# Batch 0 of a fused attention, Fourier mix and two MLPs: where the low halves of the weights, the sums of x and the first visits of batch 1 stand

## The chip, the cores and the metric

One core of a Trainium2 chip runs the whole program. The metric is the device time of one execution in microseconds (us). Before the change the median of three runs was 900.11 us (899.06 to 900.23).

## What is computed

Three layers follow one another on 4 batches of 768 tokens with 384 channels, all in float32:

```python
for t in range(S):                                   # attention layer, 8 heads of 48, per batch
    state = alpha[:, :, t, :, None] * state + einsum('bhd,bhe->bhde', k[:, :, t], v[:, :, t])
    y[:, :, t] = einsum('bhd,bhde->bhe', q[:, :, t], state)
...
u = x + real(fft(fft(x, axis=1), axis=2))            # Fourier layer, tokens then channels
un = (u - mean(u)) / sqrt(var(u) + 1e-6)
x = u + relu(un @ w_ch1) @ w_ch2                      # MLP 1: 384 -> 1536 -> 384
...
u = x + (relu(x.T @ w_tok1) @ w_tok2).T               # token mix
out = u + relu(u @ w2_ch1) @ w2_ch2                   # MLP 2
```

## The kernel before

**Numbers in two parts.** Every large product is exact to float32 by splitting each operand into a high part (a rounding copy, `fp32r`) and a low part (the difference). `three` issues high x high, high x low and low x high, at lines 1388 to 1390. A low part of an activation or a weight is a subtraction on DVE or POOL, and the high part is a copy on ACT.

**Stages.** The attention of batch 0 runs alone (`visit(0, k)`, k from -2 to 23: 4 units of two heads, 6 chunks of 128 tokens each). Its Fourier part and the first three normalised tiles follow (`tail(0, h)`, h from 31 to 47), again alone. Then the loop over b runs MLP 1 of batch b in 48 half steps h: an even h has `mlp_in` (9 matmuls of 384 columns into bank 0 or 1), an odd one `mlp_out` (9 matmuls into banks 2 to 4). Between them stand, for batch b+1, one visit in each half step up to h = 30 that isn't in `PAUSES`, and then the tail from h = 31. "MLP 0" below is this loop at b = 0. The second part of the program (token mix and MLP 2 of all batches) isn't touched.

**What a visit does.** For chunk k of batch a: PE computes the scores of chunk k+1 (L1402 in batch 0, L1406 later) and the state's product (L1415), after DVE has masked the scores before (`at`, L1049) and updated the state (`st`, L903 or L906). Then it applies `at` and the decayed state to chunk k (L1425 or L1430, L1434) and transposes the keys of chunk k+2 (L1395). DVE also prepares chunk k+3: suffix scan `suf` (L919), reciprocal, prefix scan (L931), and POOL multiplies keys and queries by them (L569, L579) and decays the state (L592). ACT copies `qz`, `krt`, `x` and `dec`. Once per unit DVE reduces the decays twice (`extreme`, L893).

**What a tail does.** `fold`: DVE adds and subtracts the two token halves of x (`x_sum`, tmp, L1054), then folds channel c with channel 384-c into xf (L1094 to L1102). `split_x` makes xh (ACT, L742) and xl (DVE, L1114). PE multiplies three flips of x (L1475), then `f1` 0 to 5, then after `split_g` (gh on ACT, gl on DVE L1118) the second transform `f2_v`, `f2_u` and `f2_middle`. `copy_flipped` (ACT, L729) and `first_edge_rows` (ACT, L734) copy the flips. From the product v, ACT makes vs (L756), DVE and POOL build u (L1127, L621, L629), and `fourier_u` (DVE, L1142) adds the product u. Statistics and un (L1193 on DVE) follow, then PE transposes un (`norm`, L1534), and nh and nl (L775, L1199) are the input of the MLP. `fill` (L1587) issues matmuls whose result nobody reads; a call of 1 shows as 2 in the trace.

**The weights.** `w_ch1` is 3 items of 128 rows (0 to 2), `w_ch2` 3 items of 4 row groups (3 to 5). Each item has two halves. The raw copies arrive on SP's queue, ACT makes the high part (`weight_hi`, L672), POOL or DVE the low one (`weight_lo`, L558 or L1278). One counter for the highs and one for the lows fix the order: before the change it is item by item. In it POOL makes halves 0 to 2 inside the attention, 3 to 5 once `xlo` is done, 6 and 7 in the first two visits of MLP 0; DVE makes 8 to 11 at h = 9, 11, 15, 17. PE waits for all of `w_ch1` before MLP 0 and for item 3 before `mlp_out(0)` at h = 5, where it also waits for all of `fourier_u` (counter `s_ua` at 10), because the result banks 2 to 4 hold Fourier products.

Nothing is planned at run time: the tables of half steps and the order of the calls in `tail` and `visit` of each engine are the whole order. Each engine runs its own list in that order, and semaphores make it wait.

Of the kernel before, what the change touches and what calls it, by code (L numbers as in the profile page):

```python
# [10 lines left out]
P = 128  # L11
# [41 lines left out]
EDGE_AT = 36  # L53
FILL_TO, FILL_COL = 5, 384
VISIT = dict(zip([h for h in range(31) if h not in PAUSES], range(-2, STEPS)))
# [9 lines left out]
LATE_NORM_AT = {9: 3, 13: 4, 20: 5}  # L65
# [25 lines left out]
def program(nc, qka, v, v_sizes, w_ch1, w_ch2, w_tok1, w_tok2, w2_ch1, w2_ch2, dft, cs, mask_in, ident_in, flip_in, col_in, out):  # L91
# [189 lines left out]

    def raw_sem(i):

        return s_raw[i % 2], 16 * (i // 2 + 1)

    def norm_bank(b, t):

        return bank[((7, 6, 4) if b == 0 else (6, 7, 6))[t] if t < 3 else 6]
# [105 lines left out]
    def f1_bank(a, i):  # L394

        return bank[5 + i % 3 if a else (5, 6, 7, 1, 5, 6)[i]]

    def v_bank(a, j):

        return bank[(5, 5, 7)[j] if a else (5, 2, 5)[j]]  # L400

    def u_bank(a, j):

        return bank[(6, 6, 5)[j] if a else (6, 3, 2)[j]]
# [15 lines left out]
    with nc.Block() as block:  # L420
# [131 lines left out]
        def _(pool):  # L552

            def weight_lo(i):
                i, half = i // 2, i % 2
                pool.wait_ge(s_whi, 2 * i + half + 1)
                src, hi, lo = halves(i, half)
                pool.tensor_tensor(lo, src, hi.bitcast(F32), ALU.subtract).then_inc(s_wlo, 1)  # L558
# [81 lines left out]
            pool.wait_ge(s_xlo, 2 * KT)  # L640
            for i in range(len(LOW_AT), LOW_F1):
                weight_lo(i)
            for a in range(B):
                if a:
                    for k in range(-2, STEPS):
                        visit(a, k)
                        if a == 1 and k < 0:
                            weight_lo(LOW_F1 + k + 2)
                fourier_v(a)
                if a:  # L650
                    fourier_v_last(a)
# [3 lines left out]
                if a == 0:  # L655
                    fourier_v_last(a)
# [9 lines left out]
        def _(act):  # L666

            def weight_hi(i):
                i, half = i // 2, i % 2
# [46 lines left out]
            def visit(a, k):  # L716
                for h in range(2 if a and (a, k) != (1, -2) else 0):
                    attn_qz(a, k + 2, h)
# [17 lines left out]
            def split_x(a, part):  # L736
                act.wait_ge(s_fold, a * 8 + (4, 8)[part])
                for i in range(part * KT, (part + 1) * KT):
                    t = f1_tile(i)
# [4 lines left out]
            def split_g(a, i):  # L744
                act.wait_ge(s_gp, a * (2 * KT) + i + 1)
                if i == 0:
                    act.wait_ge(s_fold, a * 8 + 8)
# [76 lines left out]
            for b in range(B):  # L824
                for h in range(SLOTS):
# [4 lines left out]
                    if b == 0 and h == 2:  # L830
                        for i in range(2):
                            attn_qz(1, 0, i)
# [10 lines left out]
                    if b + 1 < B:  # L843
                        if h in VISIT:
                            visit(b + 1, VISIT[h])
# [42 lines left out]
        def _(dve):  # L888
# [172 lines left out]
            def visit(a, k):  # L1061
# [11 lines left out]
                if k in (FLAG + 2, FLAG + 3):  # L1073
                    early_sum(a, k - FLAG - 2)
                if k == (FLAG - 2 if a else TEST_AT):
                    range_test(a)

            def fold(a):
# [7 lines left out]
                fold_direct(a, 0)  # L1086
                fold_rest(a, 0)
                x_sum(1, slice(EARLY, DM)).then_inc(s_xs, 1)

            def fold_direct(a, part):  # L1090

                r = slice(part * KT, (part + 1) * KT)
                dve.wait_ge(s_xs, 2 * a + part + 1)
                dve.tensor_tensor(xf[:, r, 1:192], tmp[:, r, 1:192], tmp[:, r, 383:192:-1], ALU.add).then_inc(s_fold, 1)  # L1094

            def fold_rest(a, part):
# [47 lines left out]
            def fourier_middle(a):  # L1144
# [4 lines left out]
                dve.tensor_tensor(u[0:1, 1, 0:n], bank[7][0:1, 0:n], x[0:1, 3, 0:n], ALU.add).then_inc(s_ua, 1)  # L1149
                dve.tensor_tensor(u[0:1, 1, n:DM], bank[7][0:1, n - 2:0:-1], x[0:1, 3, n:DM], ALU.add  # L1150
# [50 lines left out]

            def tail(a, h):
                if h == SUMS_AT:
                    fold(a)
                if h == SUMS_AT + 1:
                    split_x(a, 0)
                    fold_direct(a, 1)
                    split_x(a, 1)
                    fold_rest(a, 1)
                    split_x(a, 2)  # L1210
                if h == SUMS_AT + 2:
                    for i in range(KT, 2 * KT):
                        split_x(a, i)
                if 0 <= h - F1_AT < 2 * KT:
                    split_g(a, h - F1_AT)
                if h == F1_AT + 2 and a:
# [547 lines left out]
```

## Time and profile before

| | before |
|---|---|
| median of 3 runs | 900.11 us |
| the profiled execution | 900.5 us |
| its span, first to last instruction | 898.7 us |
| PE busy | 880.7 us, 98% |
| DVE busy | 456.3 us, 51% |
| ACT busy | 302.3 us, 34% |
| POOL busy | 195.8 us, 22% |
| granted TensorE clock, mean | 0.992 |

The span plus 1.8 us of start and end is the time of that execution, which is 0.4 us above the median. A granted clock of 1.00 is the 2.4 GHz level and 0.50 the 1.2 GHz level. A busy share is a mean over stages: the attention and Fourier part of batch 0 (the first 75 us) has no MLP work beside it, while from 75 us on MLP matmuls fill PE.

### The profile page before, as it was taken

The numbers are of one execution on the slowest core, as the hardware profiler recorded it, in microseconds if no ns is written. First come the engines' busy times: TensorE is split into PE (matmuls) and PEld (weight loads), VectorE is DVE, ScalarE is ACT, GpSimd is POOL, SyncE is SP. The second block draws the span as 40 slices with busy tenths as digits, with TensorE's granted clock in tenths as the row PEclk, the third lists the DMA queues.
The fourth block names the chain that finished last, engine by engine and source line by source line (L and its number), as shares of the span: only waits on it lengthen the run. The fifth ranks groups of instructions, "written<-read, shape, count | busy, mean of one in ns | idle before, by whom it ended". The sixth has DMA issues, their size and how long they took to land.

```text
span 898.7 us, 14545 instructions
## 1 busy us (share of the span) xinstructions
PE 880.7 (98%) x5378; PEld 851.5 (95%) x5378; DVE 456.3 (51%) x1085; ACT 302.3 (34%) x795; POOL 195.8 (22%) x326
## 2 busy tenths in 40 slices
PE   9996999999999999999999999999999999999998
PEld 6786999999999999999999999999999999999998
DVE  6778877658776479776552244221422142214221
ACT  2864555424544325554223242211221122112111
POOL 4754343013333023331104312000200020002000
PEclk9989999999999999999999999999999999999999
DMA  8942120040220131300054011000100010000000
GB/s 214 320 135 81 43 78 2 27 119 27 61 60 28 39 81 45 99 4 28 1 198 136 27 54 54 1 27 27 53 0 26 26 53 0 26 26 0 0 27 27
DMA packets 15002, 51.23 MB, mean 57 GB/s; under 512 B 1489, under 2 KB 6385, under 8 KB 13009
## 3 DMA queue, kind: packets, MB, share of 16 engines
q1 hardware_dynamic: 14368, 47.35, 17.4%
q0 software_dynamic: 576, 3.15, 1.0%
q8 instruction: 31, 0.51, 0.2%
q14 instruction: 27, 0.21, 0.1%
HBM read 41.07 MB, written 9.44 MB: 56 GB/s over the span
## 4 chain that ended last, share of the span: by engine, by line
PE 90%; DVE 5%; ACT 2%; issue 2%; POOL 0%; DVEq 0%; POOLq 0%
PE bank L1388 13%; PE bank L1389 13%; PE bank L1390 13%; PE pair L1388 12%; PE pair L1389 12%; PE pair L1390 12%; PE pair L1406 3%; PE bank L1425 3%; PE bank L1434 2%; PE pair L1415 2%; PE bank L1581 1%; PE bank L1534 1%; ACT tested L712 1%; PE bank L1430 1%; PE bank L1395 1%
## 5 line engine op out<-in xcount | busy, mean ns | idle before, releaser
L1255 DVE SCALAR_TENSOR_TENSOR hl<-bank,hh 128x384 fp32r<-128x384 f32 x192 | 106.8, 557 | 326.4 <-ACT hh L804 326.4
L804 ACT ACTIVATE hh<-bank 128x384 fp32r<-128x384 f32 x192 | 94.2, 491 | 352.7 <-PE bank L1390 352.7
L1388 PE MATMUL pair<-w2h,hh 128*128 128x384 f32 x288 | 101.9, 354 | 2.0 <-issue 2.0
L1388 PE MATMUL bank<-nh,w1h 128*128 128x384 f32 x288 | 102.7, 356 | 0.0
L1388 PE MATMUL bank<-u2h,w3h 128*128 128x384 f32 x288 | 96.9, 337 | 0.8 <-DVE u2l L1344 0.8
L1389 PE MATMUL pair<-w2l,hh 128*128 128x384 f32 x288 | 97.5, 338 | 0.0
L1390 PE MATMUL pair<-w2h,hl 128*128 128x384 f32 x288 | 97.4, 338 | 0.0
L1389 PE MATMUL bank<-nl,w1h 128*128 128x384 f32 x288 | 97.3, 338 | 0.0
L1388 PE MATMUL pair<-w4h,hh 128*128 128x384 f32 x288 | 97.2, 338 | 0.0
L1390 PE MATMUL bank<-nh,w1l 128*128 128x384 f32 x288 | 97.2, 337 | 0.0
L1389 PE MATMUL pair<-w4l,hh 128*128 128x384 f32 x288 | 97.0, 337 | 0.0
L1390 PE MATMUL bank<-u2h,w3l 128*128 128x384 f32 x288 | 96.5, 335 | 0.0
L1389 PE MATMUL bank<-u2l,w3h 128*128 128x384 f32 x288 | 96.5, 335 | 0.0
L1390 PE MATMUL pair<-w4h,hl 128*128 128x384 f32 x288 | 96.2, 334 | 0.0
L662 POOL TENSOR_TENSOR u<-u,x2l 128x384 f32<-128x384 f32 x24 | 23.6, 1016 | 274.9 <-DVE u L1365 274.9
L569 POOL TENSOR_TENSOR qkap<-qkap,suf 112x128 f32<-112x128 f32 (+1 forms) x81 | 39.8, 491 | 121.1 <-DVE suf L919 112.0
L686 ACT ACTIVATE qz<-qkap 48x128 f32<-48x128 f32 x144 | 44.2, 307 | 48.0 <-POOL qkap L579 45.5
L1388 PEld LDWEIGHTS pair<-w2h,hh 128*128 128x128 f32 x288 | 54.7, 190 | 2.3 <-issue 2.2
L1388 PEld LDWEIGHTS bank<-u2h,w3h 128*128 128x128 f32 x288 | 54.1, 188 | 2.1 <-issue 2.1
L1388 PEld LDWEIGHTS bank<-nh,w1h 128*128 128x128 f32 x288 | 54.8, 190 | 0.7 <-issue 0.2
L1389 PEld LDWEIGHTS bank<-nl,w1h 128*128 128x128 f32 x288 | 54.7, 190 | 0.4
L1389 PEld LDWEIGHTS pair<-w2l,hh 128*128 128x128 f32 x288 | 54.7, 190 | 0.0
(201 smaller groups left out, 1843.0 us busy)
## 6 DMA issues: line engine op xcount, KB each, us to landing
qkap<-qka SPq DMA_DIRECT2D x15, 1011.5 KB, 7.5
vt<-v SPq DMA_DIRECT2D x16, 288.0 KB, 8.0
raw_a<-w_ch SPq DMA_DIRECT2D x6, 768.0 KB, 12.1
mid<-u SPq DMA_DIRECT2D x8, 576.0 KB, 2.8
raw_b<-w_ch SPq DMA_DIRECT2D x6, 768.0 KB, 6.3
out<-u SPq DMA_DIRECT2D x8, 576.0 KB, 2.8
xr<-mid SPq DMA_DIRECT2D x7, 576.0 KB, 3.9
raw_t<-w_tok SPq DMA_DIRECT2D x2, 768.0 KB, 6.0
```

Source lines behind the costliest of these rows:

```text
L569: pool.tensor_tensor(keys.rearrange("p (c n) -> p c n", n=P), keys.rearrange("p (c n) -> p c n", n=P), after.rearrange("p (c n) -> p c n", ...
L662: pool.tensor_tensor(u2[:, t, :], u2[:, t, :], x2l[:, t, :].bitcast(F32), ALU.add).then_inc(s_u2, 1)
L686: act.activation(qz[head_rows(h), k % 2, h, :], q_of(a, k, head_rows(h)), ACT.Copy).then_inc(s_qz, 1)
L804: act.activation(hh[:, s % 4, :], bank[s % 2][:, 0:HALF], ACT.Relu).then_inc(s_hhi, 1)
L1255: dve.scalar_tensor_tensor(out=hl[:, s % 4, :], in0=bank[s % 2][:, 0:HALF], scalar=0.0, in1=hh[:, s % 4, :].bitcast(F32), op0=ALU.max, op1 ...
L1388: pe.matmul(out_ap, wh, rh, start=first, stop=False)
L1389: pe.matmul(out_ap, wh, rl, start=False, stop=False)
L1390: return pe.matmul(out_ap, wl, rh, start=False, stop=last)
L1406: return pe.matmul(score_bank(a, k)[:, 0:2 * P], k_of(a, k), qz[0:PR, k % 2, :, :].rearrange("p h t -> p (h t)"), start=True, stop=True)
L1415: return pe.matmul(kv_of(a, k), krt[:, s % 2, 0:PR], vt[unit_buffer(a, k // NC)][:, k % NC, :], start=True, stop=True)
L1425: mm = pe.matmul(y[:, h * D:(h + 1) * D], at[:, k % 2, h, :], vb[:, c, h * D:(h + 1) * D], start=h == 0, stop=c == 0 and h == 1)
L1434: mm = pe.matmul(y, q_of(a, k), dec[0:PR, k % 3, :], start=False, stop=True)
```

## The change

- The sums of x in batch 0 are made unit by unit, 6 pieces of 96 channels in visits 19 to 22, instead of two sums over 288 channels in visits 20 and 21.
- The halves of the weights are taken in another order (`WEIGHT_ORDER`): the first halves of w_ch1, then item 3, then the second halves of w_ch1. POOL makes only two lows (visits 17 and 19); DVE makes one at h = 33 of the tail and nine in MLP 0. PE's waits follow: 3 lows before MLP 0, 8 at h = 12, and 5, 10, 12 before the three parts of w_ch2.
- In MLP 0 the visits of batch 1 go from h = 5 to 30 without a pause. In MLPs 1 and 2 the pauses are 0, 1, 11, 15, 21, and the late normalisations stand at 11, 15, 21 everywhere (before: 9, 13, 20).
- The fold is cut in pieces: xf columns 1 to 127 first, then the edge columns, 128 to 254, and 256 to 383, with `split_x` between them. This holds for all batches.
- In batch 0's tail: other banks for f1, f2 and norm; ACT copies the flips and edge rows at h = 35, behind three `split_g`, instead of ahead of the first; `fill` at h = 44 is 10 instead of 6; POOL's last four products come before its preparation of batch 1; and DVE's `extreme`, prefix scan and last `fourier_u` move from the tail's end to h = 1 of MLP 0.

```diff
-PAUSES = (0, 1, 9, 13, 20)
+WEIGHT_ORDER = ((0, 0), (1, 0), (2, 0), (3, 0), (3, 1), (0, 1), (1, 1), (2, 1), (4, 0), (4, 1), (5, 0), (5, 1))
+PAUSES = ((0, 1, 2, 3, 4), (0, 1, 11, 15, 21), (0, 1, 11, 15, 21))
-FILL = {44: 6, 46: 4}
+FILL = {44: 10, 46: 4}
-HI_AT = (16, 18, 20, 21)
-HI_FOLD, HI_V, HI_MLP = 7, 10, {4: 10, 6: 11}
-LOW_AT = (17, 19, 21)
-LOW_F1 = 6
-LATE_LOW_AT = {9: 8, 11: 9, 15: 10, 17: 11}
+HI_AT = (16, 18, 20)
+HI_FOLD, HI_V, HI_MLP = 6, 9, {4: 9, 6: 10, 8: 11}
+LOW_AT = (17, 19)
+LOW_F1 = 2
+LOW_MLP = {0: (3, 4), 6: (5,), 8: (6,), 9: (7,), 10: (8,), 11: (9,), 13: (10,), 16: (11,)}
+EARLY_AT = {19: (0,), 20: (1, 2), 21: (3,), 22: (4, 5)}
-EDGE_AT = 36
+FLIPS_AT = 35
-LATE_NORM_AT = {9: 3, 13: 4, 20: 5}
+LATE_NORM_AT = {11: 3, 15: 4, 21: 5}
...
 (POOL)
-            pool.wait_ge(s_xlo, 2 * KT)
-            for i in range(len(LOW_AT), LOW_F1):
-                weight_lo(i)
...
-                if a:
-                    fourier_v_last(a)
+                fourier_v_last(a)
                 if a + 1 < B:
                     prep_k(a + 1, 0, 1)
                     prep_q(a + 1, 0, 1)
-                if a == 0:
-                    fourier_v_last(a)
 (ACT, split_x and tail)
-                act.wait_ge(s_fold, a * 8 + (4, 8)[part])
+                    act.wait_ge(s_fold, a * 10 + (2, 4, 5, 8, 10, 10)[i])
...
+                if a == 0 and h == FLIPS_AT:
+                    copy_flipped(0)
+                    first_edge_rows()
 (DVE)
+                if a == 0:
+                    for i in EARLY_AT.get(k, ()):
+                        dve.wait_ge(s_ext, 2 * NU)
+                        dve.wait_ge(s_x, NC * (i // 2 + 1))
+                        x_sum(i % 2, slice(i // 2 * PW, (i // 2 + 1) * PW))
...
                 if h == SUMS_AT + 1:
                     split_x(a, 0)
-                    fold_direct(a, 1)
+                    fold_high(a, 0)
                     split_x(a, 1)
-                    fold_rest(a, 1)
+                    late_sum(a)
                     split_x(a, 2)
+                    fold_middle(a, 1)
+                    fold_edges(a, 1)
                 if h == SUMS_AT + 2:
-                    for i in range(KT, 2 * KT):
-                        split_x(a, i)
+                    fold_low(a, 1)
+                    split_x(a, 3)
+                    fold_high(a, 1)
+                    split_x(a, 4)
+                    split_x(a, 5)
...
+                    if b == 0:
+                        for p in LOW_MLP.get(h, ()):
+                            weight_lo(p)
+                    if b == 0 and h == 1:
+                        next_unit(1)
+                        fourier_u(0, 4, 2, 0)
+                        fourier_u(0, 4, 2, 1)
 (PE)
-            pe.wait_ge(s_wlo, 2 * KT)
...
+                        if b == 0 and s in (0, NF // 2):
+                            pe.wait_ge(s_wlo, 8 if s else 3)
...
-                            pe.wait_ge(s_wlo, 2 * (KT + 1 + (s - 2) // FG))
+                            pe.wait_ge(s_wlo, {2: 5, 6: 10, 10: 12}[s])
```

First place: ACT in the tail of batch 0, from the last copy of x (`x<-bank`) to the first vs. Before the change:

```order
L692 ACTIVATE x<-bank 128x96 x2
L672 ACTIVATE w1h<-raw_a_113 128x768 x2
L672 ACTIVATE w2h<-raw_a_114 128x4x192
L742 ACTIVATE xh<-xf 128x3x128 x6
L729 ACTIVATE u_90<-pair 128x384 x3
L748 ACTIVATE gh<-pair 128x194
L748 ACTIVATE gh<-bank 128x2x192
L748 ACTIVATE gh<-bank 128x192
L734 ACTIVATE u_90<-x 1x2x384
L748 ACTIVATE gh<-bank 128x2x192
```

With the change:

```order
L693 ACTIVATE x<-bank 128x96 x2
L673 ACTIVATE w2h<-raw_a_114 128x4x192 x2
L673 ACTIVATE w1h<-raw_a_111 128x768
L743 ACTIVATE xh<-xf 128x3x128 x6
L749 ACTIVATE gh<-pair 128x194
L749 ACTIVATE gh<-bank 128x2x192
L749 ACTIVATE gh<-bank 128x192
L730 ACTIVATE u_90<-pair 128x384 x3
L735 ACTIVATE u_90<-x 1x2x384
L749 ACTIVATE gh<-bank 128x2x192
```

The three copies of the flips moved behind three `gh`, and next to the edge rows, in front of the fourth `gh`.

Second place: DVE from the end of the tail (batch 1's first suffix scan) to the first masked scores of batch 1. Before the change:

```order
L919 SCALAR_TENSOR_TENSOR suf<-qkap_57,zeros 112x128 [waits visit_done,qka_loaded0]
L925 RECIPROCAL inv<-suf 112x1 [waits suffix_done]
L893 TENSOR_REDUCE ext<-qkap_57 112x1 [waits qka_loaded0] x2
L931 SCALAR_TENSOR_TENSOR qkap_57<-qkap_57,inv,zeros 112x128 [waits inverse_ready,ext_ready]
L1142 TENSOR_TENSOR u_90<-u_90,pair 128x2x193 [waits u_done,v_added]
L1142 TENSOR_TENSOR u_90<-u_90,pair 128x2x191
L1255 SCALAR_TENSOR_TENSOR hl<-bank,hh 128x384 [waits hidden_hi] x2
```

With the change:

```order
L914 SCALAR_TENSOR_TENSOR suf<-qkap_57,zeros 112x128 [waits visit_done,qka_loaded0]
L920 RECIPROCAL inv<-suf 112x1 [waits suffix_done]
L1283 SCALAR_TENSOR_TENSOR hl<-bank,hh 128x384 [waits hidden_hi]
L1306 TENSOR_TENSOR w2l<-raw_a_114,w2h 128x4x192 [waits weight_lo,weight_hi] x2
L888 TENSOR_REDUCE ext<-qkap_57 112x1 [waits qka_loaded0] x2
L926 SCALAR_TENSOR_TENSOR qkap_57<-qkap_57,inv,zeros 112x128 [waits inverse_ready,ext_ready]
L1158 TENSOR_TENSOR u_90<-u_90,pair 128x2x193 [waits u_done,v_added]
L1158 TENSOR_TENSOR u_90<-u_90,pair 128x2x191
L1283 SCALAR_TENSOR_TENSOR hl<-bank,hh 128x384 [waits hidden_hi] x2
```

The reductions, the prefix scan and the last `fourier_u` moved behind the first `hl` and behind the two lows of item 3, which POOL made before.

## Rows read from the trace of the kernel before

**Rows 1.** The page: busy time, share of the span and instructions
```profile
PE 880.7 (98%) x5378; PEld 851.5 (95%) x5378; DVE 456.3 (51%) x1085; ACT 302.3 (34%) x795; POOL 195.8 (22%) x326
```

**Rows 2.** PE's waits, whole span: total us, times, longest
```profile
PE bank L1395 <- POOL qkap L569: 3.3, 1, 3.3
PE bank L1534 <- DVE un L1193: 2.0, 4, 1.2
PE pair L1388 <- issue: 2.0, 1, 2.0
PE bank L1430 <- DVE at L1049: 1.5, 1, 1.5
```

**Rows 3.** Stretches: width, PE busy, PEld, DVE, ACT, POOL busy, granted clock, DMA
```profile
48.30:55.20 6.90, 6.90 (x22) 5.43 (x23) 4.65 (x12) 5.14 (x10) 2.91 (x2) 0.51 0.42 133
72.10:75.00 2.90, 2.83 (x18) 2.51 (x19) 2.33 (x6) 1.75 (x5) 0.00 (x0) 1.00 0.57 155
83.20:85.70 2.50, 2.50 (x9) 2.50 (x10) 2.50 (x4) 1.21 (x4) 2.19 (x2) 0.50 0.00 0
89.40:92.60 3.20, 3.14 (x10) 3.17 (x11) 0.95 (x3) 0.62 (x2) 1.24 (x3) 0.50 0.00 0
93.90:115.40 21.50, 21.29 (x141) 20.57 (x140) 20.02 (x57) 12.86 (x40) 8.31 (x19) 1.00 0.24 63
```

**Rows 4.** DVE in order of time, visit 20: start, us, line, what
```profile
44.76 2.58 DVE L1054 TENSOR_TENSOR tmp<-x 128x864 f32<-128x864 f32 x1
```

**Rows 5.** POOL in order of time, visit 19
```profile
44.60 1.82 POOL L558 TENSOR_TENSOR w1l<-raw_a,w1h 128x768 fp32r<-128x768 f32 x1
```

**Rows 6.** ACT in order of time, tail of batch 0
```profile
53.91 1.35 ACT L742 ACTIVATE xh<-xf 128x384 fp32r<-128x384 f32 x3
...
58.25 1.23 ACT L729 ACTIVATE u<-pair 128x384 f32<-128x384 f32 x3
...
60.16 0.83 ACT L734 ACTIVATE u<-x 1x768 f32<-1x768 f32 x1
61.40 0.52 ACT L748 ACTIVATE gh<-bank 128x384 fp32r<-128x384 f32 x1 [0.41 <-PE bank L1390]
```

**Rows 7.** PE in order of time, tail of batch 0
```profile
55.74 0.55 PE L1388 MATMUL pair<-dfth,xh 128*128 128x194 f32 x1
...
63.19 0.35 PE L1388 MATMUL pair<-csh,gh 128*128 128x194 f32 x1
...
68.16 2.77 PE L1587 MATMUL bank<-mask,ident 128*128 128x256 f32 x12
72.17 0.87 PE L1534 MATMUL bank<-ident,un 128*128 128x128 f32 x6 [1.24 <-DVE un L1193]
...
74.88 0.41 PE L1388 MATMUL bank<-nh,w1h 128*128 128x384 f32 x1
```

**Rows 8.** PE in order of time, start of MLP 0
```profile
78.10 0.26 PE L1395 MATMUL bank<-ident,qkap 112*128 112x112 f32 x1
...
89.46 0.66 PE L1388 MATMUL pair<-w2h,hh 128*128 128x384 f32 x1 [2.01 <-issue]
...
115.43 0.42 PE L1388 MATMUL bank<-nh,w1h 128*128 128x384 f32 x1
```

**Rows 9.** DVE in order of time, MLP 0
```profile
75.18 1.79 DVE L893 TENSOR_REDUCE ext<-qkap 112x1 f32<-112x768 f32 x2
...
80.22 1.02 DVE L1142 TENSOR_TENSOR u<-u,pair 128x386 f32<-128x386 f32 x2 [2.72 <-POOL u L629]
...
95.16 1.45 DVE L1156 BATCH_NORM_STATS2 stats<-u 128x6 f32<-128x384 f32 x3
...
104.31 0.55 DVE L1255 SCALAR_TENSOR_TENSOR hl<-bank,hh 128x384 fp32r<-128x384 f32 x1
...
110.28 0.42 DVE L1049 TENSOR_TENSOR at<-pair,mask 128x256 f32<-128x256 f32 x1 [0.50 <-PE pair L1415]
...
111.96 0.93 DVE L1278 TENSOR_TENSOR w2l<-raw_a,w2h 128x768 fp32r<-128x768 f32 x1
```

More of the change, by code:

```diff
@@ L52 @@
 TEST_AT = 20
-EDGE_AT = 36
+FLIPS_AT = 35
 FILL_TO, FILL_COL = 5, 384
-VISIT = dict(zip([h for h in range(31) if h not in PAUSES], range(-2, STEPS)))
+VISITS = [dict(zip([h for h in range(31) if h not in pauses], range(-2, STEPS))) for pauses in PAUSES] + [{}]
 SUMS_AT = 31
@@ L552, in _, with weight_lo @@
         def _(pool):
[L554 to L557, printed above, removed]
+            def weight_lo(p):
+                pool.wait_ge(s_whi, p + 1)
+                src, hi, lo = halves(*half_at(p))
                 pool.tensor_tensor(lo, src, hi.bitcast(F32), ALU.subtract).then_inc(s_wlo, 1)
@@ L716, in visit @@
             def visit(a, k):
-                for h in range(2 if a and (a, k) != (1, -2) else 0):
+                for h in range(2 if a else 0):
                     attn_qz(a, k + 2, h)
@@ L734, in first_edge_rows, with split_x @@
                 act.activation(us[0][0:1, 3:6:2, :], x[0:1, 5:3:-1, :], ACT.Copy).then_inc(s_rows, 1)
-            def split_x(a, part):
-                act.wait_ge(s_fold, a * 8 + (4, 8)[part])
-                for i in range(part * KT, (part + 1) * KT):
-                    t = f1_tile(i)
+            def split_x(a, step):
+                for i in ((0, 1), (2,), (3, 4, 5))[step]:
+                    t, part = f1_tile(i), i // KT
+                    act.wait_ge(s_fold, a * 10 + (2, 4, 5, 8, 10, 10)[i])
                     m = slice(t * P, (t + 1) * P)
@@ L1200, in norm_split, with next_unit @@
                                   nh[:, :, cols].bitcast(F32), ALU.subtract).then_inc(s_nlo, 1)
+            def next_unit(a):
+                for i in range(2):
+                    extreme(a, 0, i)
+                prep_prefix(a, 0)
             def tail(a, h):
@@ L1245, in tail @@
                         prep_inverse(1, 0)
-                    for i in range(2):
-                        extreme(a + 1, 0, i)
-                    prep_prefix(a + 1, 0)
-                if h == 46:
+                    else:
+                        next_unit(a + 1)
+                if h == 46 and a:
                     for i in range(2):
@@ L1309, in _ @@
                         hidden(b, s)
-                    if b + 1 < B and h in VISIT:
-                        visit(b + 1, VISIT[h])
+                    if b == 0:
[5 more added lines that the diff above has]
+                        fourier_u(0, 4, 2, 1)
+                    if h in VISITS[b]:
+                        visit(b + 1, VISITS[b][h])
                     if h == LATE_STATS_AT:
@@ L1334, in _ @@
             for half in range(2):
-                weight_lo(NA + NW4, half)
+                weight_lo(2 * (NA + NW4) + half)
                 split_x2(0, half)
@@ L1338, in _ @@
             for half in range(2):
-                weight_lo(NA + NW4 + 1, half)
+                weight_lo(2 * (NA + NW4 + 1) + half)
             def split_u2(b, t):
@@ L1513, in f2_u @@
                     pe.wait_ge(s_ua, a * UA + 2)
-                elif j == 2:
+                elif j == 2 and a:
                     pe.wait_ge(s_vc, a * 3 + 2)
```

107 lines of the change are left out of this document (54 added, 53 removed).

## The prediction

> **What bounds the kernel now.** I read the page first, then PE's waits, then the stretches with the granted clock, then the timelines of the places that the change touches. PE is busy 880.7 of 898.7 us [rows 1], so a gain can only come from PE's waits and from matmuls at the low clock level. The list of waits has four places of a microsecond or more [rows 2], all ahead of 90 us: one of 1.5 us in the attention of batch 0 (masked scores from DVE), 1.2 us of the 2.0 us of un, 3.3 us in MLP 0 (POOL's keys), and 2.0 us "issue", which is PE's wait for the lows of item 3. A wait also costs clock. After the 1.5 us wait PE ran for 6.9 us at a granted 0.51 (1.2 GHz), after the 3.3 us one 2.5 us at 0.50 and after the 2.0 us one 3.2 us at 0.50; after the 1.24 us one it stayed at 1.00 [rows 3, 7]. Eighteen MLP matmuls take 78.10 - 74.88 = 3.22 us at full clock, 0.179 each [rows 7, 8]; nine are 1.6 us, and about 2.9 us at half, so a low stretch costs about 1.3 us. All in all 80 to 93 us holds some 8 us that aren't work, and 48 to 55 us another 5.
>
> **Step 1, the sums of x.** DVE's sum in visit 20 took 2.58 us [rows 4]. It had started 0.16 us after POOL's low of visit 19, which took 1.82 us [rows 5]; it ended 0.92 us after it. So DVE stood still while POOL subtracted, and PE waited 1.5 us for the scores behind [rows 2]. The change removes POOL's low of visit 21, but not this one, and puts two pieces of the sum into visit 20. They meet the same low. A piece is a third of 288 channels, about 0.4 us, and POOL's decays, which stand ahead of the low, may slip by as much behind the piece of visit 19. I take +0.3 us for the path. Afterwards the flips run on PE as before, so the earlier folds gain nothing: f1(0) starts 0.3 us later than 55.74. Bounds: -2.9 us if the pieces get through and the clock stays up, +0.5 us if two waits on POOL follow each other.
>
> **Step 2, the tail's fold and ACT.** On ACT the two last highs ahead of xh are three, as before, so xh(0) stays at about 53.9 [rows 6]. Behind it the chain is longer: the pieces stand between the xl's, and the second sum too. Counting 0.47 us for each piece of 384 elements (a fold half or an xl), 0.4 us for the sum, 0.6 us for the middle and edges, and 0.45 us for each xh [rows 6] that waits for its piece, xh(5) ends near 60.0. ACT then does three gh (0.8 us), the three flips (1.23 us) and the edge rows (0.83 us) [rows 6]: the fourth gh starts near 62.6, where it was at 61.40. Its gl and the fifth gl end near 64.05, and f2_v(0), which stood at 63.19 [rows 7], waits for them: +0.87 us. The low at h = 33 (0.93 us, as in [rows 9]) lies on DVE between two gl that wait for ACT anyway: nothing. Of the 0.87 us PE wins 0.25 back at f2_u(0), which waited before. Bounds 0 (ACT keeps up) and +1.3.
>
> **Step 3, the filler.** Twelve filler matmuls took 2.77 us, and PE then waited 1.24 us for un [rows 7]. Twenty take 4.62 us. PE arrives at 68.16 + 0.3 + 0.62 + 4.62 = 73.7; un is there at about 72.17 + 0.3 + 0.87 = 73.3. So norm starts 1.5 us later than at 72.17, and MLP 0 at 74.88 + 1.5 = 76.4. The new banks cost and bring nothing, since PE had no wait between 64.2 and 68.16.
>
> **Step 4, the first half steps of MLP 0.** DVE finishes its first suffix scan, waits for hl(0) (ready about 79.3, since mlp_in(0) ends at 78.0 and ACT and DVE take 0.5 each [rows 9]), then does two lows (2 x 0.86), two reductions (1.8), a prefix scan (0.5) and the last fourier_u (1.0) [rows 9]: 84.3. PE has done three mlp_in by 81.1 and stands before mlp_out(0), which waits for just that fourier_u. **The wait of 3.3 us is there again, with another name.** One low stretch follows, 1.3 us. What is gone is the 2.0 us for POOL's lows [rows 8] and the second low stretch, 1.3 to 1.6 us: the lows of item 3 are ready at 81.0. The wait before fourier_u (2.72 us, DVE for POOL's u [rows 9]) is gone from DVE too.
>
> **Step 5, the dense stretch.** mlp_out(0) and the first transpose take PE to about 87.6, where h = 6 begins. For h = 6 to 13 PE took 21.5 us before [rows 3]. It now has two visits more (1.3 each) and one normalisation less (0.4): 21.5 + 2.6 - 0.4 - 0.2 (the un wait) = 23.5 us. DVE was busy 20.02 us of the same stretch [rows 3]. It now has six lows in it instead of two (+3.5), two visits more (1.68 each, from the scores at 110.28 to the low at 111.96 [rows 9]: +3.4), but no statistics (1.45 and 0.45 after it [rows 9]: -1.9) and one split less (-0.5): 24.5 us. **DVE becomes the bound here**, and I count 24.7 us with the joints: PE waits about 0.5 us before the scores in h = 9, 11 and 12. That ends at 112.3. Before, PE was there at 115.43 [rows 8], with a visit and a normalisation more behind it (1.7 us). So 112.3 + 1.7 = 114.0 against 115.4: **-1.4 us**, with steps 1 to 4 in it. From h = 14 on DVE has 2.2 us a half step against PE's 2.9 and catches up.
>
> **Step 6, MLPs 1 and 2.** The late normalisation waits there for un once each, 2.0 - 1.24 = 0.8 us over three batches [rows 2, 7]; two half steps more take that away, 0.5 us outside MLP 0. In the tails of batches 1 to 3 the pieces of the fold stand on DVE with MLP matmuls over them; PE's needs come half steps later: nothing, and if the cover fails 0.3 us each.
>
> **The weights' new order** costs nothing as long as highs and lows stay ahead of PE: all second halves of w_ch1 by 100.3, needed at 106; item 4 by 107.8, needed at 109.3. That is the thinnest margin.
>
> Sum: -1.4 - 0.5 = -1.9 us. The profiled execution took 900.5 us, so 898.6; the median stood 0.4 us below it: **898.2 us**.
>
> **A rule weighed.** The 2.58 us of rows 4 is an engine that stands still for the rest of the other's instruction, not one that runs at half speed. The Trainium skill (SBUF — State Buffer, "Who interferes with whom") says that a DVE instruction with two SBUF inputs and a GpSimd instruction that reads SBUF exclude each other, and that the one issued first holds the ports to its end. By that rule POOL's low gets in ahead of a second piece wherever it was waiting, and the split gives no way past it; that is step 1 as I take it. Taken as a rate shared between both, the two pieces would end about a microsecond earlier and the sum would be near rival 1.
>
> **Rival 1, the pieces pass POOL.** If DVE keeps the ports for both pieces of visit 20, the scores come before PE asks, the 1.5 us wait and its 6.9 us at 0.51 go, and f1(0) is bound by xh instead of the flips, near 53.0. ACT's chain (step 2) gives some back: about 2.2 us better than my forecast, 896.0. For it: POOL's decays slip behind the first piece, so its low may start late. Against it: the observed order [rows 4, 5].
>
> **Rival 2, slower: DVE's lows starve the scores.** Place: h = 6 to 13. Each low also holds POOL's key and query products back, by up to its 0.93 us, and these hold the next scan and ACT's qz. If that adds 0.4 us to five half steps (+2.0) and PE's share of work there falls so far that the clock drops as it did after 1.5 us, twice at 1.4 us (+2.8), it ends at 898.2 + 4.8 = 903.0. It decides once a DVE half step with a low goes beyond about 3.4 us against PE's 2.9. For it: DVE was busy 93% of the stretch before [rows 3]. Against it: two lows were in it already and PE hardly waited.
>
> **Rival 3, nothing moves on balance.** The wait at mlp_out(0) grows to 5 us because hl(0) or the lows of item 3 come late, and eats the rest: about 900.1.
>
> **How the numbers follow.** A measurement of this kernel can tell about 0.2%, 1.8 us, from no change. Forecast 0.50, rival 1 0.22, rival 2 0.18, rival 3 0.10. The forecast's own bounds (steps 1 to 3, +-1.3 us) put a bit more than half of it below 898.3: 0.28 faster and 0.22 same. With rival 1 faster is 0.50, with rival 3 and a hundredth of rival 2 same is 0.33, slower 0.17. The range reaches from the middle of rival 1 (895.0, with its clock gain in full) to 901.6, which takes in rival 3 and the light end of rival 2.
>
> **What would show it.** Step 1: two tmp pieces in visit 20, the second over 1 us long, and PE's wait of about 1.5 us for `at` still in the list, with a clock of 0.5 until 55. Step 2: f2_v(0) waits for gl. Step 4: no "issue" wait of 2 us, but one of about 3.3 us before the first `pair<-w2h`, behind fourier_u, and one low stretch after it, not two. Step 5: DVE over 95% busy for some 25 us, and several waits of PE for `at` below 1 us. It is wrong if PE's total wait between 75 and 115 us falls below 2 us or stays over 8 us, or if the clock between 48 and 55 us is up.

## The result and the profile after

The changed kernel is slower: 901.83 us median of 8 runs (901.26 to 902.92), where the kernel before took 899.7 us beside it. The ratio is 1.0033, with a 95% interval of 1.002 to 1.0046, so the loss is 3.0 us. Medians are over all runs, a few of which took 912 to 920 us in a slower state that any of these kernels can fall into; the ratios, and the comparisons drawn below, leave those out. My prediction was 898.2 us with a range of 895.0 to 901.6, so it missed on the sign and, by 0.2 us, on the range.

| | before | after |
|---|---|---|
| the profiled execution | 900.5 us | 902.67 us |
| its span | 898.7 us | 900.9 us |
| PE busy | 880.7 us | 883.0 us |
| f1 of batch 0 begins | 55.74 | 56.35 |
| f2_v of batch 0 begins | 63.19 | 64.62 |
| MLP 0 begins | 74.88 | 76.32 |
| its first mlp_out | 89.46 | 84.37 |
| mlp_in of h = 14 | 115.43 (with a visit and a normalisation more behind it) | 114.07 |
| mlp_in of h = 24 | 143.30 | 144.11 |

From f1 on the rows are the start times, in us, of the first matmul named. At h = 24 both kernels have done the same number of visits and normalisations, so there the balance of batch 0 can be read: 0.81 us lost.

These two executions did not start alike. PE in order of time (start, us, line), first of the kernel before, then of the changed one:

```profile
1.48 8.36 PE L1581 MATMUL bank<-at 128*128 128x384 f32 x16 [1.48 <-DVE ones L1282]
9.67 0.26 PE L1395 MATMUL bank<-ident,qkap 112*128 112x112 f32 x1
...
38.95 0.41 PE L1415 MATMUL pair<-vt,krt 128*112 128x96 f32 x2 [0.45 <-ACT krt L679]
```

```profile
1.47 7.12 PE L1614 MATMUL bank<-at 128*128 128x384 f32 x16 [1.47 <-DVE ones L1310]
8.43 0.26 PE L1428 MATMUL bank<-ident,qkap 112*128 112x112 f32 x1
...
38.05 0.41 PE L1448 MATMUL pair<-vt,krt 128*112 128x96 f32 x2 [0.45 <-ACT krt L680]
```

The 16 matmuls ahead of the first product took 8.36 us in one and 7.12 us in the other, and 0.9 us of that difference is still there at 38 us. It isn't the change's: a second trace with the kernel before's code up to this point (the variant with the pauses moved, below) has 7.11 us there and stands at 38.02. So whoever subtracts one of these traces from the other finds the changed kernel 0.9 us better in batch 0 than it is. Added to the 2.2 us between the two spans, it comes near the 3.0 us of the ratio.

The page of the changed kernel, busy time by engine, answers to [rows 1]:

```profile
PE 883.0 (98%) x5386; PEld 853.1 (95%) x5386; DVE 461.4 (51%) x1103; ACT 303.6 (34%) x795; POOL 184.5 (20%) x320
```

PE's waits over the span (total us, times, longest us) answer to [rows 2]:

```profile
PE pair L1421 <- DVE u L1158: 3.1, 1, 3.1
PE pair L1439 <- ACT qz L687: 3.1, 3, 1.2
PE bank L1463 <- DVE at L1044: 1.5, 1, 1.5
PE pair L1439 <- DVE st L901: 0.7, 1, 0.7
PE bank L1421 <- DVE gl L1134: 0.6, 1, 0.6
```

The wait for POOL's keys and the "issue" wait are gone, and the wait for un with them. The 3.1 us for the last fourier_u and the 1.5 us for the masked scores are those I had forecast. The second line had 0.4 us before: three waits for ACT's qz. One of 0.77 us stands in MLP 0. The other two are in no step of my working. They are the next two rows, at half step 9 of MLP 1 and of MLP 2:

```profile
230.50 0.67 PE L1439 MATMUL pair<-qz,qkap 112*128 112x256 f32 x2 [1.17 <-ACT qz L687]
...
355.72 0.67 PE L1439 MATMUL pair<-qz,qkap 112*128 112x256 f32 x2 [1.18 <-ACT qz L687]
```

ACT in order of time, at the first of the two, shows what qz stands behind:

```profile
229.12 0.71 ACT L771 ACTIVATE un<-u,nrm 128x384 f32<-128x384 f32 x1 [2.02 <-DVE nrm L1202]
229.73 0.62 ACT L687 ACTIVATE qz<-qkap 48x128 f32<-48x128 f32 x2
```

ACT sits idle for 2.02 us in front of un, because DVE's Newton steps for the late normalisation end only at 229.08; qz comes behind un on the same queue. The kernel before has the same pair of ACT instructions with the same 2.02 us of idle time:

```profile
228.47 0.71 ACT L770 ACTIVATE un<-u,nrm 128x384 f32<-128x384 f32 x1 [2.02 <-DVE nrm L1186]
...
229.09 0.63 ACT L686 ACTIVATE qz<-qkap 48x128 f32<-48x128 f32 x2
```

It had a pause at half step 9, so PE had no visit there and asked for no qz. The change moves the pauses to 11, 15 and 21 and puts a visit exactly there.

### The profile page after: what moved, and what is told of

Read it like the earlier page. It is cut to its first block, busy times and chain, and to the rows that moved or that the text cites. A ratio compares the mean times of both kernels' runs of the same rounds, so it can differ in the third digit from the quotient of the medians.

```text
span 900.9 us, 14589 instructions
## 1 busy us (share of the span) xinstructions
PE 883.0 (98%) x5386; PEld 853.1 (95%) x5386; DVE 461.4 (51%) x1103; ACT 303.6 (34%) x795; POOL 184.5 (20%) x320
## 4 chain that ended last, share of the span: by engine, by line
PE 88%; DVE 4%; ACT 3%; issue 2%; DMA 1%; SPq 0%; POOL 0%; DVEq 0%; ACTq 0%
PE bank L1421 13%; PE bank L1422 13%; PE bank L1423 13%; PE pair L1421 12%; PE pair L1422 12%; PE pair L1423 12%; PE pair L1439 3%; PE bank L1458 3%; PE bank L1467 2%; PE pair L1448 1%; DMA qkap<-qka 1%; PE bank L1567 1%; ACT tested L713 1%; PE bank L1463 1%; PE bank L1428 1%
```

## The experiments

Each time is a median, each ratio is to the kernel before, measured beside it on the same chip, with its 95% interval. The runs of the kernel before spread over 896.8 to 901.2 us, so that single microseconds are read from the trace and the sum from the ratio.

**Pauses back.** In MLPs 1 and 2 alone, of the changed kernel:

```
-PAUSES = ((0, 1, 2, 3, 4), (0, 1, 11, 15, 21), (0, 1, 11, 15, 21))
+PAUSES = ((0, 1, 2, 3, 4), (0, 1, 9, 13, 20), (0, 1, 9, 13, 20))
-LATE_NORM_AT = {11: 3, 15: 4, 21: 5}
+LATE_NORMS = [{11: 3, 15: 4, 21: 5}] + [{9: 3, 13: 4, 20: 5}] * 3
```

> The changed kernel with the pauses of MLPs 1 and 2 and their late normalisations back at 9, 13, 20. Theory A, the half step h = 9 without a pause costs: ACT copies qz of the next visit behind the un that waits for DVE's Newton steps, and PE stood 1.17 and 1.18 us for it at 230.5 and 355.7 us, where the kernel before stood 0.30 and 0.27 us for un. Undone, the two waits go and the old ones return: 1.8 us faster than the changed kernel, about 900.0 us, 1.0013 of the kernel before. Theory B, the two waits only move within MLPs that DVE or ACT bound anyway: no difference, 1.0033 of the kernel before.

Measured: 899.72 us, ratio 1.0011 (1.0001 to 1.002), against 1.0033 of the changed kernel. Both qz waits are gone and the two of 0.3 us for un are back. By the ratios about two thirds of the loss lie here (2.0 of 3.0 us; the two intervals just meet at 1.002).

**The pauses alone, in the kernel before.**

```
+PAUSES_12 = (0, 1, 11, 15, 21)
-VISIT = dict(zip([h for h in range(31) if h not in PAUSES], range(-2, STEPS)))
+VISITS = [dict(zip([h for h in range(31) if h not in p], range(-2, STEPS))) for p in (PAUSES, PAUSES_12, PAUSES_12)] + [{}]
-LATE_NORM_AT = {9: 3, 13: 4, 20: 5}
+LATE_NORMS = [{9: 3, 13: 4, 20: 5}] + [{11: 3, 15: 4, 21: 5}] * 3
```

> The kernel before with one part of the change alone: in MLPs 1 and 2 the pauses at half steps 11, 15 and 21 and the late norms there, batch 0 as before. My theory (ACT's qz stands behind un, which waits for DVE's Newton steps, 0.9 us at h = 9 of each of two MLPs): slower by 1.8 us, ratio 1.002, and PE's chain shows two waits of about 1.2 us for qz near 229 and 354 us where 0.3 us for un stood. Rival (the forecast's own term: 0.5 us gained): ratio 0.9994. Second rival (the waits of the changed kernel came from its batch 0, by the phase at which batch 1 begins): ratio 1.000, no qz waits.

Measured: 901.21 us, ratio 1.0027 (1.0015 to 1.0039), slower, where no other part of the change is present. PE in order of time shows the same two waits:

```profile
226.82 0.67 PE L1407 MATMUL pair<-qz,qkap 112*128 112x256 f32 x2 [1.17 <-ACT qz L687]
...
352.18 0.67 PE L1407 MATMUL pair<-qz,qkap 112*128 112x256 f32 x2 [1.18 <-ACT qz L687]
```

Removing the part takes 2.0 us away by the ratios, adding it alone costs 2.4 us, and the trace has 1.8 us for it. The largest part of the loss is settled from both sides, and my forecast's own term (0.5 us gained) and the phase of batch 1 both fall.

**Sums of x whole again** (visits 20 and 21, as before):

```
-                if a and k in (FLAG + 2, FLAG + 3):
+                if k in (FLAG + 2, FLAG + 3):
-                if a == 0:
-                    for i in EARLY_AT.get(k, ()):
...
-                        x_sum(i % 2, slice(i // 2 * PW, (i // 2 + 1) * PW))
```

> The changed kernel with the sums of x whole again, 288 channels in visits 20 and 21; POOL's lows stay at visits 17 and 19. Theory A, the piece of visit 19 is what costs: DVE stood in it for 3.49 us behind four POOL instructions, the scores of chunk 21 came that late, and PE then ran 10.1 us at the low clock level instead of 6.9. Undone, DVE meets only POOL's second low, the low stretch falls back to about 7 us, f1(0) starts 1.2 us earlier against the attention: 1.2 us faster than the changed kernel, about 900.6. Theory B, only the number of POOL instructions counts and any sum there waits as long: no difference.

Measured: 900.61 us, ratio 1.0016 (1.0005 to 1.0026); this overlaps the changed kernel's interval. The profile of the same kernel is read from one more execution, of 901.67 us:

> The changed kernel with the sums of x whole again in batch 0 (visits 20 and 21, as before), looked at for its profile. My theory: no DVE instruction of a 0.45 us size then stands 3.49 us behind four GpSimd instructions; DVE's tmp in 41 to 47 us takes at most 2.5 us, the un wait and the wait at 46 us are gone or under 0.6 us, and f1 of batch 0 begins 0.5 to 1.5 us earlier than 56.35. Rival (the piece costs nothing, the clock alone differs between executions): f1 begins at 56.0 to 56.6 again, and a wait of 1 us or more stands at 44 to 47 us with the whole sums too. Time about 900.6.

DVE, POOL and PE of the changed kernel in order of time, around the piece of visit 19, first:

```profile
42.30 3.49 DVE L1049 TENSOR_TENSOR tmp<-x 128x288 f32<-128x288 f32 x1
...
46.27 0.81 DVE L1049 TENSOR_TENSOR tmp<-x 128x288 f32<-128x288 f32 x2
...
41.15 1.82 POOL L567 TENSOR_TENSOR w1l<-raw_a,w1h 128x768 fp32r<-128x768 f32 x1
42.95 0.76 POOL L601 TENSOR_SCALAR dec<-st,suf 48x48 f32<-48x48 f32 x2
43.68 1.79 POOL L567 TENSOR_TENSOR w1l<-raw_a,w1h 128x768 fp32r<-128x768 f32 x1
...
46.27 1.14 PE L1463 MATMUL bank<-vt,at 128*128 128x96 f32 x4 [1.46 <-DVE at L1044]
```

And the same engines with whole sums:

```profile
44.12 2.55 DVE L1049 TENSOR_TENSOR tmp<-x 128x864 f32<-128x864 f32 x1
...
43.94 1.81 POOL L567 TENSOR_TENSOR w1l<-raw_a,w1h 128x768 fp32r<-128x768 f32 x1
45.73 1.20 POOL L601 TENSOR_SCALAR dec<-st,suf 48x48 f32<-48x48 f32 x1
...
47.63 0.66 PE L1458 MATMUL bank<-vt,at 128*128 128x96 f32 x4 [1.47 <-DVE at L1044]
```

A piece of 0.4 us takes 3.49 us: it starts while POOL's first low runs and ends 0.3 us after the second, with two decays between them. The four other traces with this code in this place have 3.50 to 3.54 us. Two pieces with no low beside them take 0.81 us together. The whole sum waits only for one low: it got in directly behind it, and it was POOL's decay that took 1.20 us there instead of 0.39. But my theory of the price falls: PE's wait is still 1.47 us, one visit later. The rival had the wait right, and f1 wrong: it is 2.6 us earlier (53.71 against 56.35), and what differs there is the clock: after its 1.47 us wait this execution stayed at 1.00. Rows of stretches (width, busy time of PE, PEld, DVE, ACT, POOL, granted clock, DMA), changed kernel:

```profile
48.00:52.00 4.00, 4.00 (x19) 3.50 (x20) 1.80 (x6) 0.93 (x4) 0.54 (x1) 0.50 0.61 207
52.00:56.00 4.00, 4.00 (x9) 2.50 (x8) 2.81 (x8) 3.29 (x7) 0.00 (x0) 0.50 0.04 12
```

Whole sums, and there a low stretch further on, behind a wait of 1.67 us for gl at 62.92:

```profile
48.00:52.00 4.00, 3.33 (x20) 2.45 (x20) 2.67 (x8) 2.23 (x6) 0.94 (x1) 1.00 0.64 207
52.00:56.00 4.00, 3.52 (x20) 2.67 (x19) 2.87 (x8) 2.00 (x4) 0.00 (x0) 1.00 0.01 4
...
64.00:68.00 4.00, 4.00 (x25) 3.78 (x24) 3.46 (x10) 1.23 (x3) 0.45 (x1) 0.57 1.05 303
```

Of the 2.6 us little is left at MLP 0, which begins at 76.18 against 76.32: f2_v waits for DVE's gl (ACT's chain) and the clock falls there instead.

**No low on POOL in the attention.** All three of POOL's lows come after the last xl; none on DVE at h = 33:

```
-LOW_AT = (17, 19)
-LOW_F1 = 2
+LOW_AT = ()
+LOW_F1 = 3
...
-                    if a == 0 and h == F1_AT:
-                        weight_lo(LOW_F1)
...
+            pool.wait_ge(s_xlo, 2 * KT)
+            for i in range(LOW_F1):
+                weight_lo(i)
```

> The changed kernel with no low of the weights in the attention: POOL makes the first three once xlo is done, DVE none at h = 33. The sums stay in pieces. Theory A, the 1.5 us wait and the low clock level from 46 to 56 us come from DVE standing behind POOL's lows: the scores of chunk 21 and 22 are in time, PE runs at 1.00, and f1(0) starts when xl(0) is ready, some 2.5 us earlier: about 899.3. Theory B, the wait is DVE's own work (sums and range test): no more than 0.5 us is gained. A loss would mean that three lows, 5.4 us on POOL, delay its Fourier products.

Measured: 899.69 us, ratio 1.0003 (0.9991 to 1.0014), about 2.7 us under the changed kernel by the ratios, as theory A had it. The 1.5 us wait is gone and the clock stays up to 80 us. The profiled execution (897.85 us) is one of the quick ones of a spread from 897.3 to 901.0, and the gain is handed on like this in it (PE in order of time):

```profile
51.36 0.36 PE L1422 MATMUL pair<-dfth,xh 128*128 128x194 f32 x1
...
60.57 0.36 PE L1422 MATMUL bank<-csh,gh 128*128 128x194 f32 x1 [1.68 <-DVE gl L1137]
...
72.62 0.41 PE L1422 MATMUL bank<-nh,w1h 128*128 128x384 f32 x1
80.67 0.69 PE L1422 MATMUL pair<-w2h,hh 128*128 128x384 f32 x1 [3.13 <-DVE u L1161]
```

f1 is 5.0 us earlier than in the changed kernel, f2_v 4.1 and MLP 0 3.7: ACT's chain and the filler take the rest.

**The last fourier_u ahead of the first hl:**

```
-                        next_unit(1)
-                        fourier_u(0, 4, 2, 0)
-                        fourier_u(0, 4, 2, 1)
+                        next_unit(1)
...
+                    if b == 0 and h == 0:
+                        fourier_u(0, 4, 2, 0)
+                        fourier_u(0, 4, 2, 1)
```

> The changed kernel with the last two fourier_u ahead of the first hl on DVE, where DVE stood idle for 1.82 us, instead of behind two lows, two reductions and the prefix scan. Theory A, PE's 3.13 us wait ahead of mlp_out(0) and the 6.1 us at the low clock level behind it come from this order alone: both go, mlp_out(0) starts near 81.1, DVE's idle 2.8 us near 90 us goes too, and the time falls by about 4 us, to 897.8. Theory B, DVE bounds the whole stretch up to 114 us: the wait only moves into the visits behind, and less than 1.5 us is gained.

Measured: 898.96 us, ratio 1.0001 (0.999 to 1.0012), 2.9 us under the changed kernel where I expected 4. The 3.13 us wait and the low stretch behind it are gone. Part of them comes back as two waits for DVE, of which the first is new and the second was 0.26 us before; two more, of 0.64 and 0.76 us, stood there before too:

```profile
85.88 0.45 PE L1422 MATMUL bank<-nh,w1h 128*128 128x384 f32 x1 [0.72 <-DVE hl L1283]
91.30 0.67 PE L1440 MATMUL pair<-qz,qkap 112*128 112x256 f32 x2 [1.26 <-DVE st L898]
```

**Two smaller ones.** The flips of batch 0 on ACT four half steps earlier (`copy_flipped(0)` at SUMS_AT + 2 in place of FLIPS_AT), and the filler back from ten to six:

```
-FILL = {44: 10, 46: 4}
+FILL = {44: 6, 46: 4}
```

> The changed kernel with ACT's three copies of the flips back ahead of the first gh of batch 0 (behind the third xh), where ACT waits for the fold anyway. Theory A, they hold the fourth gh back and with it f2_v(0), for which PE stood 0.65 to 1.66 us: the wait shrinks to at most 0.2, everything behind follows, 0.8 us faster than the changed kernel (901.8), 1.0024 of the kernel before. Theory B, the filler and DVE's path to un set the end, not f2_v(0): less than 0.3 us.

Measured: 900.7 us, ratio 1.0016 (1.0004 to 1.0028). The trace bears theory A out. The kernel with the pauses back has the changed kernel's code in batch 0, and f1 began at 55.37 there and at 55.39 here, so these two can be compared. PE's rows for f2_v, first with the flips late, then with the flips early:

```profile
64.57 0.35 PE L1421 MATMUL bank<-csh,gh 128*128 128x194 f32 x1 [1.61 <-DVE gl L1134]
```

```profile
63.74 0.36 PE L1422 MATMUL bank<-csh,gh 128*128 128x194 f32 x1 [0.73 <-DVE gl L1135]
```

ACT's fourth gh starts at 61.88 instead of 63.18, f2_v 0.83 us earlier, and MLP 0 at 75.44 instead of 76.26: all of it is handed on. The wait shrank to 0.73 us, not to the 0.2 I expected. By the times it is 1.5 us under the changed kernel, in overlapping intervals.

> The changed kernel with 6 instead of 10 fillers at h = 44. Theory A, un is ready when the last filler ends (the last un at about 73.7 against a filler end at 73.6), so the fillers cost nothing: no change within 0.3 us, and PE shows a wait for un of about 1 us at full clock. Theory B, the fillers are 0.5 us too many: 0.4 us faster. A loss of 1 us or more would mean that the clock falls in that wait, which is what the fillers guard against.

Measured: 901.54 us, ratio 1.0027 (1.0015 to 1.0039): no change that can be told. A wait of 0.7 us for un stands where eight matmuls of filler were, and the clock behind it stays at 1.00, as with the fillers.

**All four edits together** (pauses, fourier_u, lows, flips), and then with lows 3, 4 and 5 of the MLP's weights on POOL, between its two preparations of the first chunk of batch 1, instead of on DVE:

> The changed kernel with four edits of before together: old pauses in MLPs 1 and 2, the last fourier_u ahead of the first hl, no POOL low in the attention, flips early. If the places are independent their gains add: 2.0 + 2.9 + 2.7 from the timed runs and 0.8 for the flips, 8 us and more off 901.8, to about 893.5, 0.993 of the kernel before. If two of them share one low clock stretch or the DVE bound of MLP 0 takes back what comes early, 895.5 or more.

Measured: 894.33 us, ratio 0.9956 (0.994 to 0.9971), 6.9 us under the changed kernel by the ratios. The single gains add up to 8.4, so it lies between the two theories and tells neither from the other.

```
-LOW_MLP = {0: (3, 4), 6: (5,), 8: (6,), 9: (7,), 10: (8,), 11: (9,), 13: (10,), 16: (11,)}
+POOL_MLP = (3, 4, 5)
+LOW_MLP = {8: (6,), 9: (7,), 10: (8,), 11: (9,), 13: (10,), 16: (11,)}
...
                     prep_k(a + 1, 0, 1)
+                    if a == 0:
+                        for p in POOL_MLP:
+                            weight_lo(p)
                     prep_q(a + 1, 0, 1)
```

> As the four edits together, and POOL makes the two lows of item 3 and the first second half of w_ch1 while it has nothing to do between its key and query products of chunk 0 (idle for 6.1 us), instead of DVE at h = 0 and h = 6. Theory A, DVE bounds PE up to h = 13 of MLP 0 (PE waited 1.26, 0.72, 0.64 and 0.76 us for DVE's or its followers' work there): three lows less are 2.7 us of DVE, and 1.5 to 2.5 us come off against the four edits, to about 891.5. Theory B, PE isn't held by DVE's work but by the order of the chain: under 0.7 us. POOL's lows, 5.4 us, could also hold DVE's scan; then no gain.

Measured: 894.13 us, ratio 0.9941 (0.9919 to 0.9962). The intervals of the two overlap, so no gain is shown, and 891.5 is not reached. The waits for hl and st of 0.7 and 1.3 us are gone, but a low stretch stands behind a wait of 2.5 us for un that both kernels have. The same six transposes, first with the four edits, then with POOL's lows:

```profile
70.90 0.87 PE L1570 MATMUL bank<-ident,un 128*128 128x128 f32 x6 [2.52 <-DVE un L1213]
```

```profile
71.28 1.51 PE L1574 MATMUL bank<-ident,un 128*128 128x128 f32 x6 [2.50 <-DVE un L1217]
```

The granted clock from 72 to 74 us is 1.00 in the first trace and 0.50 in the second.

**A pause at 9 and the norms at 11.** The last kernel, with its pauses in MLPs 1 and 2 at 9, 15, 21 and late norms at 11, 15, 21 (`PAUSES = ((0, 1, 2, 3, 4), (0, 1, 9, 15, 21), (0, 1, 9, 15, 21))`):

> The kernel e8 (four parts of the change undone or moved, lows of the MLP on GpSimd) with pauses of MLPs 1 and 2 at 9, 15, 21 and all late norms at 11, 15, 21. My theory (what costs is a visit at h = 9, beside ACT's un; the later norms themselves save the 0.25 us un waits): 0.5 us under e8, about 893.6, ratio 0.9935, no qz wait of over 0.9 us at half step 9. Rival (the late norm itself at 11 puts ACT's un ahead of a qz again): qz waits of 1 us move to half step 11, 1 to 2 us over e8, about 895.5.

Measured: 892.77 us (892.67 to 892.92), ratio 0.9931 (0.991 to 0.9951). Between 200 and 450 us PE waits for nothing any more: it is the visit at 9 that costs, not the later normalisation. The two waits for un of 0.3 us, which I had hoped to gain, are gone and no wait for qz has come for them; the times alone can't tell this kernel from the last one (0.9931 and 0.9941, with intervals that overlap). This is the fastest version, some 6 us under the kernel before and 9 under the changed one.

**The third low back on DVE**, with two on POOL, in the kernel with POOL's lows in the MLP:

> The kernel e8, but with two lows on GpSimd behind xlo and the third (the last half of the fold's weights) on VectorE as in the changed kernel. My theory: the 2.5 us wait of the norm of batch 0 for DVE's un in e8 came of the third low on GpSimd, that its Fourier products stand behind; here that wait is under 1 us and the time is 1 to 2 us under e8, about 892.5, ratio 0.992. Rival (GpSimd isn't what un waits for; ACT's or DVE's own order is): the wait stays at 2 to 2.6 us and the time within 0.5 us of e8, or above it by the 1 us of the low on DVE.

Measured: 897.13 us, ratio 0.9977 (0.9966 to 0.9988), 3.2 us above that kernel by the ratios. DVE, POOL and PE in order of time, in the version with the pause at 9, which has the same code in batch 0 as that kernel (three lows on POOL):

```profile
60.86 2.63 DVE L1151 TENSOR_TENSOR u<-x,vs 128x193 f32<-128x193 f32 x2 [1.09 <-ACT vs L764]
63.41 1.27 DVE L1151 TENSOR_TENSOR u<-u,vs 128x193 f32<-128x193 f32 x2
...
57.25 5.43 POOL L568 TENSOR_TENSOR w1l<-raw_a,w1h 128x768 fp32r<-128x768 f32 x3 [10.81 <-DVE xl L1138]
62.69 1.19 POOL L631 TENSOR_TENSOR u<-x,vs 128x193 f32<-128x193 f32 x2
63.84 1.23 POOL L631 TENSOR_TENSOR u<-u,vs 128x193 f32<-128x193 f32 x2
...
71.03 1.51 PE L1574 MATMUL bank<-ident,un 128*128 128x128 f32 x6 [2.51 <-DVE un L1217]
```

And with two on POOL and one on DVE:

```profile
60.96 0.96 DVE L1314 TENSOR_TENSOR w1l<-raw_a,w1h 128x768 fp32r<-128x768 f32 x1 [3.52 <-POOL w1l L568]
...
65.60 0.63 DVE L1151 TENSOR_TENSOR u<-x,vs 128x193 f32<-128x193 f32 x2 [1.95 <-ACT vs L764]
66.14 0.62 DVE L1151 TENSOR_TENSOR u<-u,vs 128x193 f32<-128x193 f32 x2
...
63.44 0.53 PE L1430 MATMUL bank<-csh,gh 128*128 128x194 f32 x1 [4.42 <-DVE gl L1142]
```

The un wait is gone, and without POOL beside them the four products take 1.25 us instead of 3.9. But this doesn't show that they were the 2.5 us of the wait. From f2_v to the first un it is 11.0 us with three lows on POOL and 9.8 us here, 1.2 us less. The rest is PE's: behind the new wait of 4.42 us its clock was 0.50 to 69 us, and from f2_v to the filler it took 7.4 us instead of 4.6. The edit put that wait in: the low on DVE waits for POOL's second low (lows are counted in order), and four gl stand behind it. Both sides of the expectation are half right, and its time was wrong by 4.6 us for a queue that I had not read.

## Why the prediction was wrong

- **Step 6 failed, by 2.3 us.** It said "two half steps more take that away, 0.5 us outside MLP 0". I had looked at the norms' new place, and not at what the pauses' old place was good for. It measured +1.8 us in the trace (2.35 us of qz waits less the 0.57 of un), and 2.0 and 2.4 us by the ratios of the two kernels with one edit. The rows for the qz waits were there in the trace of before: ACT's 2.02 us idle ahead of un at half step 9, and qz behind it. Step 6 doesn't make the sign alone: with the pauses back the ratio is still 1.0011, above one, where steps 1 to 5 promised 1.4 us gained. In the tails, where the step put nothing, a wait of 0.2 to 0.3 us for xl ahead of f1 is gone in each of three batches, which brought PE 0.5 us forward in all.
- **Step 5 was off by 2.2 us.** h = 6 began at 87.48 (forecast 87.6), h = 14 at 114.07 (112.3): 1.8 us. DVE is the bound, 20.91 of 22 us busy, with waits of 0.26, 0.67 and 0.77 us, near those described, the last one for ACT's qz. The other 0.4 us are the work that the kernel before still had to do at h = 14: I put 1.7 us on a visit and a normalisation, and by h = 24 it took 2.17. Of the 1.8 us about 1.2 are the low clock, which step 4 had ended too early: "one low stretch, 1.3 us" was two groups of nine matmuls, mlp_out(0) and the mlp_in of h = 6. Stretches of the changed kernel:

```profile
84.00:88.00 4.00, 3.63 (x12) 3.54 (x13) 3.88 (x13) 0.70 (x3) 0.87 (x2) 0.50 0.00 0
88.00:92.00 4.00, 4.00 (x19) 3.93 (x18) 1.15 (x5) 1.47 (x5) 0.00 (x0) 0.72 0.00 0
94.00:116.00 22.00, 20.56 (x135) 19.28 (x134) 20.91 (x53) 12.86 (x41) 10.88 (x21) 1.00 0.16 46
```

 With the pauses back and with the whole sums, two other executions of the same code in this place, it was one group, and h = 14 began at 112.89 and 112.80. So the size of this part wasn't to be had from one trace, and 0.5 us of the stretch stay without a cause.
- **Step 1 had its number by luck.** The flips began 0.30 us later than before (53.30 against 53.00), the 0.3 us I took, but only because the changed kernel's execution had started 0.9 us ahead. Counted from PE's row at 38 us the flips begin after 14.05 and 13.64 us in the two traces with the code of before, and after 15.25, 14.81 and 14.78 us in three with the changed code (the changed kernel, the pauses back, fourier_u first): 0.7 to 1.6 us later. The mechanism was another too. No piece of visit 20 met the low; the piece of visit 19 did, behind four POOL instructions. The low stretch lasted from 46.0 to 56.1, not 6.9 us as in [rows 3], which made f1 0.6 us late. The rule of the Trainium skill that I had weighed (SBUF — State Buffer, "Who interferes with whom": the instruction issued first holds the ports to its end) fits the whole sum, which ended behind one low, and names the direction for the piece. The traces go beyond it: the piece was passed over by three further POOL instructions, in all five of them. Rival 1, in which the pieces pass POOL, fell.
- **Steps 2, 3 and the waits of step 4 were right, with some luck in step 2.** f2_v came 0.82 us later behind f1 (forecast 0.87), waiting for gl. ACT's chain sets its time, whenever f1 comes: with the pauses back f1 began at 55.37 and f2_v at 64.57, which is 1.75 us later behind f1, so the 0.82 fits because f1 was late. Norm found un ready, MLP 0 began at 76.32 (76.4), the first mlp_out at 84.37 (84.3) after 3.13 us for the last fourier_u, and no "issue" wait.
- **Rival 2** had the sign, but its mechanism isn't what made the kernel slower: behind the waits of h = 8 to 13 the clock did not fall (1.00 from 94 to 116 us), and all waits of h = 6 to 13 are 1.7 us. Rival 3 comes near batch 0's number, 0.81 us lost, but not by its mechanism: the wait at mlp_out(0) was 3.13 us and not 5.
- The sum of the trace is 0.8 + 1.8 - 0.5 = 2.1 us, and the two profiled executions differ by 902.67 - 900.5 = 2.17. With the 0.9 us by which they started apart it is about the 3.0 us of the ratio.

## What to carry to other kernels

When work is moved into a slot that was kept free, ask first what the empty slot was covering: look in the old trace at that very place for an engine's idle time with the moved work's producer queued behind it, on every engine that the work passes. When a wait of PE is removed, follow the gain through the next two dependent chains before counting it; here ACT's chain and the filler took 1.3 of 5.0 us before MLP 0 began. Before a small instruction is put beside a stream of another engine's, ask what it costs if it waits for several of these and not for one. And before two traces are subtracted, compare them at a point that the change can't have touched.

## What was not expected of the hardware

- **A waiting DVE instruction is let in between POOL's in one place and not in another.** A 0.4 us subtraction took 3.49 us, through the rest of one low, two decays and another low, and 3.50 to 3.54 us in four more traces. The whole sum got in directly behind its low. So did the first of the four products in the tail, 2.04 us long, which ended 0.2 us behind POOL's third low though POOL went on with products of its own; the other three took 0.67 us each:

```profile
60.86 2.04 DVE L1151 TENSOR_TENSOR u<-x,vs 128x193 f32<-128x193 f32 x1 [1.09 <-ACT vs L764]
```

 What decides it stays open.
- **The clock after a wait isn't a function of the wait.** Behind the wait of 2.5 us for un it stayed at 1.00 with the four edits and fell to 0.50 until about 74 us in the two kernels that followed, whose code up to there is the same. After the wait of 1.5 us for the masked scores TensorE ran at 0.50 until 56.1 in the changed kernel, and stayed at 1.00 with whole sums, with f1 2.6 us apart. In the kernel before f1 began at 55.74, and at 53.81 in its variant with the pauses moved, whose code up to there is the same; 0.9 us of that was there at 38 us, the rest is the clock (0.60 against 0.92 in 52 to 56 us). The spread of the runs does not go with this wait either: with no low on POOL in the attention the wait was gone, and the runs still spread over 897.3 to 901.0 us. What makes the spread stays open.
